# RWKV, soft MoE and feed-forward in one kernel: TensorE's turning of tokens moved from the end of a step to between its scores and its outputs

## The reference

```python
# attention: 4 batches, 8 heads, 768 positions, head size 48, all float32
for t in range(S):
    cur = np.einsum('bhd,bhe->bhde', u[None] * kt, vt)     # the bonus
    y[:, :, t] = np.einsum('bhd,bhde->bhe', rt, state + cur)
    state = w[None, :, :, None] * state + np.einsum('bhd,bhe->bhde', kt, vt)
# x = y laid out as 3072 tokens by 384
logits = x @ phi                                    # 384 x 32 slots
d = softmax of logits over the tokens; slot_input = d.T @ x
slot_out = expert MLPs with relu (8 experts, 4 slots each, 384 -> 1024 -> 384)
x = softmax of logits over the slots @ slot_out
h = x @ w_in                                        # 384 -> 2048
out = (h * sigmoid(1.702 * h)) @ w_out              # 2048 -> 384
```

## Time and profile before

| what | value |
|---|---|
| median of 3 runs | 404.63 us (403.53 to 405.27) |
| time of the profiled execution | 403.24 us |
| its span | 401.4 us |
| PE busy | 387.7 us, 97% of the span |
| DVE busy | 234.8 us, 58% |
| ACT busy | 188.1 us, 47% |
| POOL busy | 111.7 us, 28% |
| PE's share of the chain that ended last | 89% |
| mean granted clock of PE | 0.987 |

### The profile page before, as it was taken

One profiled execution on the slowest core, in us unless ns is written; L12 is line 12 of the kernel. 1 busy time (PEld: TensorE's weight loads), 2 busy tenths in 40 slices (PEclk: granted clock), 3 DMA queues, 4 the chain that ended last, 5 costly groups with the idle time before them and its releaser, 6 DMA issues.

```text
span 401.4 us, 9106 instructions
## 1 busy us (share of the span) xinstructions
PE 387.7 (97%) x3234; PEld 308.1 (77%) x3234; DVE 234.8 (58%) x423; ACT 188.1 (47%) x432; POOL 111.7 (28%) x113
## 2 busy tenths in 40 slices
PE   4879999999999999999999999999999999999996
PEld 4768888888887744577888888888888888888885
DVE  7667777777778220148565655556565555656551
ACT  1053444444443413376656445554654555456452
POOL 5678777777755021015330000000000000000000
PEclk9599999999999999999999999999999999999999
DMA  7799999999999969980002000200010020002002
GB/s 236 281 376 397 347 327 308 324 321 320 324 301 356 373 214 379 410 293 2 1 0 78 2 0 2 78 0 0 15 63 0 0 78 0 0 0 78 2 0 78
DMA packets 28613, 63.89 MB, mean 159 GB/s; under 512 B 2640, under 2 KB 16576, under 8 KB 28208
## 3 DMA queue, kind: packets, MB, share of 16 engines
q1 hardware_dynamic: 27600, 63.12, 44.2%
q10 hardware_dynamic: 992, 0.49, 0.6%
HBM read 58.88 MB, written 4.72 MB: 158 GB/s over the span
## 4 chain that ended last, share of the span: by engine, by line
PE 89%; DMA 4%; DVE 2%; SPq 1%; issue 1%; POOL 1%; ACT 1%; DVEq 0%; POOLq 0%
PE bank L569 16%; PE bank L571 16%; PE bank L570 16%; PE bank L329 5%; PE bank L360 5%; PE bank L354 5%; PE bank L556 5%; PE bank L347 3%; PE bank L381 3%; PE bank L495 3%; PE bank L476 3%; DMA krb<-kr 2%; DMA rkb<-rk 2%; PE bank L372 2%; PE bank L390 2%; PE bank L404 1%
## 5 line engine op out<-in xcount | busy, mean ns | idle before, releaser
L794 DVE TENSOR_TENSOR gf<-bank,sg 128x512 f32<-128x512 f32 x96 | 66.3, 692 | 86.2 <-ACT sg L945 85.8
L569 PE MATMUL bank<-glo,whi 128*128 128x512 f32 x288 | 112.4, 390 | 0.2 <-DVE glo L800 0.2
L571 PE MATMUL bank<-ghi,wlo 128*128 128x512 f32 x288 | 112.1, 389 | 0.0
L570 PE MATMUL bank<-ghi,whi 128*128 128x512 f32 x288 | 112.0, 389 | 0.0
L945 ACT ACTIVATE sg<-bank 128x512 f32<-128x512 f32 x96 | 57.3, 598 | 93.9 <-PE bank L556 93.9
L800 DVE TENSOR_TENSOR glo<-gf,ghi 128x512 fp32r<-128x512 f32 x96 | 69.4, 723 | 0.2
L569 PEld LDWEIGHTS bank<-glo,whi 128*128 128x128 f32 x288 | 54.1, 188 | 12.3 <-DVE glo L800 1.2
L571 PEld LDWEIGHTS bank<-ghi,wlo 128*128 128x128 f32 x288 | 54.1, 188 | 11.3
L570 PEld LDWEIGHTS bank<-ghi,whi 128*128 128x128 f32 x288 | 54.1, 188 | 11.1
L951 ACT ACTIVATE ghi<-gf 128x512 fp32r<-128x512 f32 x96 | 59.9, 624 | 0.9 <-DVE gf L794 0.9
L837 ACT ACTIVATE yt<-bank 112x512 f32<-112x512 f32 x24 | 14.3, 598 | 65.0 <-PE bank L360 65.0
(11 more groups left out here) (121 smaller groups left out, 390.1 us busy)
## 6 DMA issues: line engine op xcount, KB each, us to landing
ring<-w SPq DMA_DIRECT2D x24, 512.0 KB, 5.8
rkb<-rk SPq DMA_DIRECT2D x23, 512.0 KB, 5.0
krb<-kr SPq DMA_DIRECT2D x24, 384.0 KB, 5.2
ring<-w SPq DMA_DIRECT2D x4, 1536.0 KB, 13.9
ring<-w SPq DMA_DIRECT2D x8, 768.0 KB, 10.7
vb<-v SPq DMA_DIRECT2D x24, 192.0 KB, 5.1
out<-ob SPq DMA_DIRECT2D x18, 256.0 KB, 2.1
ring<-win SPq DMA_DIRECT2D x3, 1024.0 KB, 14.1
```

The costliest lines, as they stand in the source:

```text
L569: pe.matmul(o, w_hi, lo, start=(f == 0), stop=False)
L570: pe.matmul(o, w_hi, hi, start=False, stop=False)
L571: pe.matmul(o, w_lo, hi, start=False, stop=(f == KF - 1)).then_inc(prod_ps, 1)
L794: dve.tensor_tensor(gf[:, f % 2, :], bank[f % 4][:, :], sg[:, f % 2, :], ALU.mult).then_inc(gf_ok, 1)
```

## The change

In a step, `tokens(n-2)` on PE now stands directly behind `scores(n)` and before the transposes of `vd`. `turns(c-1)` moves from the step with b = 1 to the step with b = 2, behind `tokens`. ACT copies the bank YN by one operation of 128x384 instead of two of 128x192, for which each transpose writes at a distance of 128 columns instead of 112; `yn_ok` counts one per step. On ACT `rows(n-2)` now stands before `columns(n-1)`, except with b = 2, where it stays behind `decay`; `turned(c-1)` stands first in the step with b = 2. The calls behind the 24 steps keep their order.

```diff
--- before.py
+++ after.py
@@ -376,9 +376,9 @@
             def tokens(c, b):
                 n = B * c + b
                 wait(pe, yt_ok, n + 1)
-                wait(pe, yn_ok, 2 * n)
+                wait(pe, yn_ok, n)
                 for hp in range(HP):
-                    last = pe.transpose(YN[:, hp * PAIR:(hp + 1) * PAIR], yt[0:PAIR, b, hp, :],
+                    last = pe.transpose(YN[:, hp * P:hp * P + PAIR], yt[0:PAIR, b, hp, :],
                                         idt[0:PAIR, 0:PAIR])
                 last.then_inc(yn_ps, 1)
 
@@ -399,7 +399,7 @@
 
             def gather(c):
                 wait(pe, tr_ok, 2 * (c + 1))
-                wait(pe, yn_ok, 2 * (B * c + B))
+                wait(pe, yn_ok, B * c + B)
                 for b in range(B):
                     last = pe.matmul(LG[32 * b:32 * b + 32, 0:DM], eg[:, 32 * b:32 * b + 32],
                                      yn[:, b, :, :, :].rearrange("p a i e -> p (a i e)"), start=True, stop=True)
@@ -413,15 +413,16 @@
                     logits(c - 1)
                 scores(c, b)
                 if not is_first(c, b):
+
+                    if not is_first(*prev(c, b)):
+                        tokens(*prev(*prev(c, b)))
+                    if tail and b == 2:
+                        turns(c - 1)
                     outputs(*prev(c, b))
                     if b == 0 or not is_last(c):
                         state(*prev(c, b))
-                    if tail and b == 1:
-                        turns(c - 1)
                     if tail and b == 2:
                         gather(c - 1)
-                    if not is_first(*prev(c, b)):
-                        tokens(*prev(*prev(c, b)))
 
             pe.wait_ge(s_phi, 16)
             steps(pe, step)
@@ -850,10 +851,9 @@
                 act.wait_ge(yn_ps, n + 1)
                 if b == 0:
                     wait(act, p_ps, c)
-                for i in range(2):
-                    act.activation(yn[:, b, :, i, :],
-                                   YN[:, 0:HP * PAIR].rearrange("p (h e) -> p h e", h=HP)[:, :, 64 * i:64 * i + D],
-                                   ACT.Copy).then_inc(yn_ok, 1)
+                act.activation(yn[:, b, :, :, :],
+                               YN[:, :].rearrange("p (h i e) -> p h i e", h=HP, i=2)[:, :, :, 0:D],
+                               ACT.Copy).then_inc(yn_ok, 1)
 
             def exponentials(c):
                 act.wait_ge(lt_ps, c + 1)
@@ -879,12 +879,15 @@
                 if is_last(c) and b == 3:
                     row_exp(0, EARLY)
                 if not is_first(c, b):
+                    turning = not is_first(*prev(c, b))
+                    if tail and b == 2:
+                        turned(c - 1)
+                    if turning and b != 2:
+                        rows(*prev(*prev(c, b)))
                     columns(*prev(c, b))
                     if not is_last(prev(c, b)[0]):
                         decay(*prev(c, b))
-                    if tail and b == 1:
-                        turned(c - 1)
-                    if not is_first(*prev(c, b)):
+                    if turning and b == 2:
                         rows(*prev(*prev(c, b)))
 
             def high_weights(which, t):
```

## The result

The changed kernel takes 407.36 us (median of 11 runs, 406.02 to 408.78), the kernel before 405.02 us on the same chip (11 runs, 403.53 to 405.92). The ratio is 1.0066 with a 95% interval of 1.0051 to 1.0082: slower by 2.1 to 3.3 us. The profiled execution took 408.05 us with a span of 406.3.

The account below looks back on a forecast made before the run. PE was taken as the bound, with loops through DVE and ACT close behind. Four middle chunks at +1.1 and the last chunk at +1.7 gave +2.8 us: 403.24 to 406.0 profiled, median 407.4, range 404.0 to 409.0.

Parts of the forecast that it names:

- PE's saving of 0.14 a step: Steps 2 to 23: tokens behind the scores cost PE 0.39 instead of 0.53 us, 3.1 us in all.
- b = 3: Middle chunks, step with b = 3: scores wait for DVE's scaling, released 0.39 later; +0.05 us.
- b = 1: Middle chunks, step with b = 1: tokens and turns leave, tokens come in, DVE decides at 4.63; -0.17 us.
- b = 2: Middle chunks, step with b = 2: tokens and turns come in, the gather covers DVE; +0.08 us, so 5.45.
- b = 0: Step with b = 0: logits wait for ACT's delayed copy of YT, 4.89 instead of 4.58 into the step; +0.31 us.
- Step 21: Last chunk, b = 1, no state products behind it: DVE's 4.63 decides instead of PE's 4.52; +0.11 us.
- The row maximum: Last chunk, b = 2: DVE's row maximum waits for later turned copies, holding up mask, scaling and next scores; +0.9 us.
- The end of step 23: Last step, b = 3: tokens, formerly free within the wait for YT's copy, now precede it; +0.39 us.
- The first chunk's steps: First chunk: PE idles over a microsecond before scores, behind loads, which hides either place of tokens; counted as nothing.
- The first rival: The loops through DVE and ACT don't bind and PE's whole saving shows: -3.1 us, 401.5; chance 0.07.
- The second: Rival: loops bind but the last chunk's row maximum hides: +2.0 us or less, 406.0 to 406.6; chance 0.23.
- The third: Rival: copy of YN with b = 2 comes too late for next tokens: +1.0 to +2.5 on top; chance 0.12.

Follow-up runs that it names:

- e4: The changed kernel with four buffers for the scaled rks instead of two; 404.78 us, ratio to the kernel before 1.001.
- e1: The kernel before, order unchanged, with only the single ACT copy of 128x384 and the 128-column distance between transposes; 404.74 us, ratio 0.9999.
- e5: The kernel before, order unchanged, with four buffers for the scaled rks; 404.68 us, ratio 1.0012.
- e7: The changed kernel with the last chunk's turns back in the step with b = 1; 406.19 us, ratio to the kernel before 1.0045.
- e2: The changed kernel with tokens behind the state products again in steps with b = 0; 405.28 us, ratio to the kernel before 1.0031.
- e6: The changed kernel with four rks buffers, tokens behind state products with b = 0 and in step 23, last chunk's turns with b = 1; 402.29 us, ratio to before 0.9952.

## Why the prediction was right

The mechanism was as forecast: PE does have less to do, and three waits that tokens used to cover cost more than that. The median rose by 2.34 us against a forecast of 2.8 (406.0 from 403.24), the ratio says 2.1 to 3.3; the stretch that the sum was about grew by 2.74. That the forecast for the median, 407.4, was met by 407.36 is luck: it started from 404.63, and the kernel before had 405.02 beside the changed one. Point by point:

- PE's saving of 0.14 a step: shown by the 4.44 of e4.
- b = 3, forecast +0.05: measured +0.03. b = 1, -0.17: -0.17. b = 2, +0.08: +0.07. The first two rested on the release of rks moving by 0.39, which DVE's rows show to the hundredth.
- b = 0, forecast +0.31: +0.27. I took 0.09 from ACT's end to PE's start, from the one row that had it; here it was 0.05.
- A middle chunk therefore +0.20 instead of +0.27, and four of them +0.8 instead of +1.1.
- The written-out last chunk: step 20 +0.27. Step 21 +0.20 instead of +0.11, since PE began 0.14 behind DVE's end (125.34 to 125.48), and the same made step 19 last 4.73. The 0.06 came from one row and holds in the loop; the written-out steps take more. I also took the 4.52 of the kernel before for PE's own time; e1 and e5 have 4.44.
- The row maximum, forecast +0.9 (or +0.75 with DVE's operations overlapping): +0.82, and e7 shows the cause. Here two errors cancel: DVE's operations do overlap (from L680 to L662 0.73 and from there to the scaling 1.24, where I added 0.82 and 1.34), and the scores start 0.14 instead of 0.06 after the scaling.
- The end of step 23, forecast +0.39: +0.40.
- The first chunk's steps count as nothing: no run shows otherwise. Its profile is 2.05 us late there, but e1 and e5 show the same in the old order. Step 4 lasts 5.97 instead of 5.86 in the changed profile, 0.11 that I hadn't in the sum; it is the low clock at its start.
- The loads, taken as 0: from step 4 on neither PE nor DVE waits for one. In step 3 DVE does wait for one, 1.29, but it does so in the old order as well.

The errors are of both signs and cancel in the stretch: 0.3 too much in the middle chunks and 0.1 in the row maximum, 0.1 too little in each of the steps 4, 19 and 21. That 2.74 lies as near 2.8 as it does is therefore in part luck; that each wait binds, and for about how long, is not. The first rival (waits that don't bind) fails by the idle times and by e4. The second (the row maximum hides) fails by 5.82. The third (the copy of YN late with b = 2) didn't happen; its cover was 0.25, a little more than the 0.1 to 0.2 counted. Tiling and drains: the saving of 0.14 us for one group less a step agrees with the Trainium skill's rule that a mode switch drains the engine (TensorEngine Tiling (Array Packing), Key Properties). No run separates the drain from whatever else a change of group costs, and the rule alone would have given the wrong sign.

## What to carry to other kernels

An engine that is busy for 100% of a stretch still has loops through other engines running close behind it. Before moving work on it from behind a release to in front of it, measure the slack of each loop: from the release to the start of what waits, through to where the busy engine needs it again. Where the moved work is longer than the slack (0.39 against 0.34 and 0.08 here), that step gets longer by the difference, although the busy engine does less; where it is shorter, the step gains, as with b = 1 here. And the group that seems to cost time at the end of a step may be what covers a wait: move it together with the buffer, or the input, that makes the wait go away; count the consumer's own program order too, where one late input (of the row maximum here) holds up everything that stands behind it.

## What the runs showed of the hardware

- The first steps scatter by up to 2.1 us between executions, in the same order of work: scores of step 4 at 30.44 (before), 32.41 (e1) and 32.31 (e5) in the old order, 30.43 (e4) to 32.49 (changed) in the new. Where they are late (31.51 and more), PE worked in step 3 at a granted clock of 0.50 to 0.67, after 2.04 to 3.26 us of idle time; in the kernel before and in e4 it had 1.18 and 1.67 us of idle time there and a clock of 1.00; e2, with 2.44 us and a clock of 0.66, began step 3 early enough (25.50) to reach step 4 at 30.59. The scatter is about as much as that of the runs of one kernel (2.4 us before, 2.8 us changed, in the first comparison).
- From an end on DVE to the start of the waiting scores it is 0.05 to 0.06 us in the loop and 0.14 to 0.16 in the written-out steps; from ACT's end to PE 0.05 before the logits (in the loop and in the written-out step 20 alike) and 0.09 to 0.10 before the last vd transposes. No run shows why they differ.
- From step 5 on the kernels repeat themselves to about 0.01 us a step from profile to profile, so terms of 0.03 us can be read from a single profile while the whole time scatters by 2 us. The two exceptions found are steps that DVE's own work held up: step 21 of the kernel before (4.52, where e1 and e5 have 4.44) and one of 4.50 among those of 4.44 in e6.
